# Two softmax products cut in halves, and weight blocks, softmax steps and loads at other places, in an attention, expert-FFN and routing kernel on one core

## The reference

```python
# attention: x (4, 8, 512, 64), state (4, 8, 32, 64)
scores  = scale * x @ state.T ;  a  = softmax(scores);   xread = a  @ state     # 512 rows a batch and head
scores2 = scale * state @ x.T ;  a2 = softmax(scores2);  sread = a2 @ x         # 32 rows a batch and head
x = concat([xread, sread], axis=2) -> (2176, 512)
# FFN: w_in (512, 2048), w_out (2048, 512)
h = x @ w_in ;  g = h * tanh(softplus(h)) ;  x = g @ w_out
# routing to 8 experts: logits = normalised x @ normalised expert_emb.T / tau
out[rows of expert e] = gate * (relu(x @ w1[e]) @ w2[e])
```

## Time and profile before

| | |
|---|---|
| median of three executions | 699.39 us (699.05 to 701.37) |
| the profiled execution: its own time | 701.31 us |
| the profiled execution: span, first to last instruction | 699.5 us |
| PE busy | 657.1 us, 94% of the span |
| DVE busy, ACT busy | 442.5 us, 385.9 us |
| granted PE clock, mean | 0.983 of full speed |

### The profile page before, as it was taken

How to read it: one execution, slowest core, us unless ns; L and a number is a source line. 1 busy time by engine, 2 the same in 40 slices (tenths; PEclk the granted TensorE clock), 3 DMA queues, 4 the chain that set the end, 5 groups by cost and what they waited for, 6 DMA issues and landing times.

```text
span 699.5 us, 12384 instructions
## 1 busy us (share of the span) xinstructions
PE 657.1 (94%) x4142; PEld 513.4 (73%) x4143; DVE 442.5 (63%) x687; ACT 385.9 (55%) x501; POOL 50.8 (7%) x75
## 2 busy tenths in 40 slices
PE   7889979999989999899999999889999999999995
PEld 5667657687767787676578877678888888888883
DVE  6899889979548699685677658462722452262261
ACT  2789678785547887477787453252622442261250
POOL 1000000000200002000000103001001010010101
PEclk9999999999989999999999999999999999999998
DMA  9713453000814000344000531472621360153140
GB/s 264 218 32 107 151 166 121 0 2 2 269 45 135 37 2 31 95 137 154 9 1 8 219 106 77 162 261 76 220 82 45 109 211 30 45 197 134 45 150 5
DMA packets 35350, 72.72 MB, mean 104 GB/s; under 512 B 5699, under 2 KB 5699, under 8 KB 35312
## 3 DMA queue, kind: packets, MB, share of 16 engines
q1 hardware_dynamic: 27728, 56.93, 25.3%
q0 software_dynamic: 3040, 9.13, 3.3%
q10 hardware_dynamic: 4544, 6.14, 2.9%
HBM read 60.92 MB, written 12.16 MB: 104 GB/s over the span
## 4 chain that ended last, share of the span: by engine, by line
PE 64%; DVE 16%; ACT 10%; issue 5%; DMA 4%; SPq 0%; ACTq 0%; POOL 0%; DVEq 0%; POOLq 0%
PE PS L708 16%; PE PS L736 16%; PE PS L613 11%; PE PS L569 7%; DVE ww L1384 3%; PE PS L717 3%; PE PS L524 3%; DMA raw<-in_w 2%; PE PS L478 2%; ACT ww L981 2%; DVE qq L1396 2%; ACT rr L977 2%; DVE qq L1379 2%; DVE gl L1402 2%; ACT rr L975 1%
## 5 line engine op out<-in xcount | busy, mean ns | idle before, releaser
L613 PE MATMUL PS<-WH,gh 128*128 128x512 f32 x256 | 103.3, 404 | 0.8 <-DVE gl L1402 0.8
L613 PE MATMUL PS<-WH,gl 128*128 128x512 f32 x256 | 101.0, 395 | 0.0
L613 PE MATMUL PS<-WL,gh 128*128 128x512 f32 x256 | 101.0, 394 | 0.0
L1067 ACT ACTIVATE hh<-PS 128x512 fp32r<-128x512 f32 x42 | 23.0, 596 | 96.4 <-PE PS L717 94.3
L736 PE MATMUL PS<-WH,hh 128*128 (+1 forms) x168 | 68.6, 409 | 3.1 <-DVE hl L1488 2.0
L1478 DVE TENSOR_TENSOR WL<-raw,WH 128x1024 f32 (+1 forms) x48 | 56.2, 1222 | 23.5 <-ACT WH L1047 23.4
L736 PE MATMUL PS<-WH,hl 128*128 (+1 forms) x168 | 66.5, 396 | 0.0
L736 PE MATMUL PS<-WL,hh 128*128 (+1 forms) x168 | 66.2, 394 | 0.0
L1379 DVE SCALAR_TENSOR_TENSOR qq<-ww,PS 128x1024 f32<-128x1024 f32 (+1 forms) x35 | 41.5, 1187 | 35.5 <-ACT ww L965 35.4
L981 ACT ACTIVATE ww<-ww,cst 128x1024 f32<-128x1024 f32 (+1 forms) x35 | 39.4, 1127 | 41.6 <-DVE ww L1384 41.6
L613 PEld LDWEIGHTS PS<-WH,gh 128*128 128x128 f32 x256 | 48.2, 188 | 18.8 <-issue 7.5
(11 more groups left out here) (252 smaller groups left out, 1281.8 us busy)
## 6 DMA issues: line engine op xcount, KB each, us to landing
raw<-in_w SPq DMA_DIRECT2D x48, 512.0 KB, 4.6
raw<-in_w_in SPq DMA_DIRECT2D x36, 512.0 KB, 4.9
yg<-by_expert ACTq DMA_DIRECT2D x22, 260.0 KB, 3.4
raw<-in_w_out SPq DMA_DIRECT2D x8, 512.0 KB, 4.6
by_expert<-junk SPq DMA_DIRECT2D x1, 2080.0 KB, 10.2
wr<-in_w_in SPq DMA_DIRECT2D x4, 512.0 KB, 9.4
x_0a<-in_x SPq DMA_DIRECT2D x8, 128.0 KB, 3.0
x_0b<-in_x SPq DMA_DIRECT2D x8, 128.0 KB, 3.6
```

The source lines that it names most:

```text
L613: mm = pe.matmul(PS[:, 2 + t, :], a[:, v % 2, e, t * P:t * P + P], w[:, 8 + p, e * 512:e * 512 + 512], start=(p == 0 and e == 0 and i == 0 ...
L1067: a.activation(hh[:, 4 * j:4 * j + 4, :], PS[:, 3 + j, :].rearrange("p (k m) -> p k m", k=4), ACT.Copy).then_inc(hh_rdy, 1)
```

## The change

It does six things.

1. `sread(1)`, `sread(2)` and `sread(3)` are cut in two: the products of t in `ahead` and `behind`, with the work of H or Y between the two halves. `sread(0)` stays whole.
2. In `sread(2)` and `sread(3)` the products of the two head groups g alternate, g = 1 writes a bank of its own (7) and another 32 partitions (q = j xor 1), so that eight parts of the array are used in turn instead of four. The reciprocal of the sums is written to the partitions that fit (five small DVE instructions instead of one), and `sread_out` needs two copies instead of four.
3. The blocks M(c+1, 1) and M(c+1, 2) of chunks 1 and 2 go to other pairs, M(c+1, 3) goes into the next chunk, and `M_hi`, `M_lo` with them, some of these between other steps of mish.
4. `scores_out`, `soft_1`, `soft_3`, `soft_4`, `exp_1` and `soft_5` of batches 2 and 3 go one pair or a few steps ahead.
5. In chunk 0, pair 5, ACT does `exp_1(1)` ahead of `sread_out(0)`, and `o_split(6)` behind the exponentials of mish.
6. In SP's queue `load_x(2)` goes behind four more weight loads, and `load_x(3)` behind four more.

```diff
             sp.dma_start(scr_v[0:PAD], ...).then_inc(zeros_out, 16)
+            for r in range(12, 16):
+                stream(r)
             load_x(2)
-            for r in range(12, RING["w", 2 * NB, 0]):
+            for r in range(16, RING["w", 2 * NB + 2, 0]):
                 stream(r)
             load_x(3)
...
-            def sread(b):
+            def sread(b, part):
                 pe.wait_ge(e2d_rdy, b + 1)
                 if b > 1:
-                    pe.wait_ge(m_lo, NB * b + 1)
+                    pe.wait_ge(m_lo, NB * b + 2)
...
+                order = [(g, t) for g in range(HG) for t in range(16)] if b < 2 else [(g, t) for t in range(16) for g in range(HG)]
+                for g, t in order[part]:
+                    for j in range(4):
+                        q = j if b < 2 else j ^ g
+                        mm = pe.matmul(PS[32 * q:32 * q + 32, sr_bank(b, g), D * g:D * g + D], E2D[b][32 * j:32 * j + 32, g, 32 * t:32 * t + 32],
+                                       X2[b % 2][t // 8][32 * j:32 * j + 32, g, t % 8, :],
+                                       start=(t == 0), stop=(t == 15))
+                if part.stop is None:
+                    mm.then_inc(sr_mm, 1)
...
+            whole, ahead, behind = slice(0, None), slice(0, 16), slice(16, None)
...
                     if p == 4:
+                        if c == 1:
+                            sread(1, behind)
                         route_k(c - 1)
+                    if p == 6:
+                        sread(c + 1, ahead)
+                    if p == 7:
+                        sread_turned(c + 1)
+                if c > 1 and p == 0:
+                    M(c, 3)
...
                     if p == 3 and c == 1:
-                        sread(1)
+                        sread(1, ahead)
                     if p == 5 and c > 0:
-                        sread(c + 1)
+                        M(c + 1, 1)
                     if p == 6 and c > 0:
-                        sread_turned(c + 1)
+                        sread(c + 1, behind)
                     if p == 7:
-                        M(c + 1, 3)
+                        M(c + 1, 3 if c == 0 else 2)
...
                 if u == 5:
+                    exp_1(1)
                     sread_out(0)
-                    exp_1(1)
-                    o_split(6)
...
-                if n == 4 and c in (1, 2):
+                if n == 3 and c in (1, 2):
                     exp_1(c + 1)
```

More of the change, by code:

```diff
@@ L267, in h_bank, with sr_bank, sh_upto, bv_upto @@
             return 6 if v == 1 else 0
+        def sr_bank(b, g):
+            return 6 if b < 2 else 6 + g
+        def sh_upto(b):
+            return (4, 8, 10, 12)[b]
+        def bv_upto(b):
+            return (2, 4, 10, 16)[b]
         def y_bank(t):
@@ L758, in _ @@
                     if p == 4:
-                        sread(0)
+                        sread(0, whole)
                 if c in (1, 2):
@@ L930, in sread_out @@
                 for h in range(2):
-                    for g in range(HG):
-                        a.activation(sh[D * h:D * h + D, 2 * g:2 * g + 2, NS * b:NS * b + NS], ps[:, g, :, h if g == 0 else 1 - h, :],
+                    if b < 2:
+                        for g in range(HG):
+                            a.activation(sh[D * h:D * h + D, 2 * g:2 * g + 2, NS * b:NS * b + NS], ps[:, g, :, h if g == 0 else 1 - h, :],
+                                         ACT.Copy).then_inc(sh_e, 1)
+                    else:
+                        a.activation(sh[D * h:D * h + D, :, NS * b:NS * b + NS].rearrange("p (g q) n -> p g q n", g=HG), ps[:, :, :, h, :],
                                      ACT.Copy).then_inc(sh_e, 1)
@@ L1085, in _ @@
                 mish_b(u)
+                if u == 6:
+                    o_split(6)
                 if u < PC - 1:
@@ L1120, in _ @@
                     mish_hi(u - 1)
+                if n == 7 and c in (1, 2):
+                    M_hi(c + 1, 1)
                 if done >= 0:
@@ L1140, in _ @@
                     exp_2(1)
+                if n == 6 and c in (1, 2):
+                    M_hi(c + 1, 0)
+                if n == 2 and c in (1, 2):
+                    scores_out(c + 1)
                 if done >= 0 and n == 1:
                     y_out(done)
+                    if c > 1:
+                        M_hi(c, 2)
                 mish_c(u)
+                if c == 1 and n == 0:
+                    M_hi(1, 2)
                 if done >= 0:
@@ L1326, in soft_5 @@
                 v.tensor_scalar(r2[:, b % 2, 2, :], r2[:, b % 2, 2, :], 1e-9, None, ALU.add).then_inc(bv, 1)
-                dve.wait_ge(bv, 2 * b + 1)
-                v.reciprocal(r2[:, b % 2, 3, :], r2[:, b % 2, 2, :]).then_inc(bv, 1)
+                if b < 2:
+                    dve.wait_ge(bv, bv_upto(b) - 1)
+                    v.reciprocal(r2[:, b % 2, 3, :], r2[:, b % 2, 2, :]).then_inc(bv, 1)
+                else:
+                    dve.wait_ge(bv, bv_upto(b) - 5)
+                    v.reciprocal(r2[:, b % 2, 3, 0:1], r2[:, b % 2, 2, 0:1]).then_inc(bv, 1)
+                    for j in range(4):
+                        q = j ^ 1
+                        v.reciprocal(r2[32 * q:32 * q + 32, b % 2, 3, 1:2], r2[32 * j:32 * j + 32, b % 2, 2, 1:2]).then_inc(bv, 1)
                 v.transpose(E2D[b][:], SC[:]).then_inc(e2d_rdy, 1)
@@ L1612, in _ @@
                     mish_lo(u - 1)
-                if kind == "m" and n < 3 and c > 0:
+                if n == 7 and c in (1, 2):
+                    M_lo(c + 1, 1)
+                if kind == "m" and (n in (0, 2) and c == 1 or n == 2 and c > 1):
                     M_lo(c, n + 1)
-                if n == 7 and c in (1, 2):
-                    M_lo(c + 1, 0)
                 if c == 1 and n == 0:
@@ L1624, in _ @@
                 mish_r(u)
+                if n == 6 and c in (1, 2):
+                    M_lo(c + 1, 0)
+                if n == 1 and c > 1:
+                    M_lo(c, 2)
                 if done >= 0 and n == 1:
@@ L1627, in _ @@
                 mish_g(u)
+                if n == 0 and c > 1:
+                    sread_scale(c)
+                if c == 1 and n == 0:
+                    M_lo(1, 2)
                 if c in (1, 2):
```

47 lines of the change are left out of this document (15 added, 32 removed).

## The result

Median 688.42 us over 4 runs (686.82 to 692.68), 700.38 us before on the same chip, 12.0 us less; the ratio is 0.985, 95% interval 0.981 to 0.989. The forecast was 686.9 us, range 683.5 to 691. The profiled execution took 686.94 us with a span of 685.2 us, of which PE was busy for 651.3 (95%); the forecast for it was a span of 687.0 us.

What follows compares the result with a forecast made beforehand. PE, busy 94% of the span, was taken as the bound, with time to win in idle and slow time at four places. 2.5 + 1.35 + 6.05 + 2.45 + 1.0 - 0.8 = 12.55 us, giving 686.9 us, range 683.5 to 691.

Steps and rivals of the forecast that it cites:

- Place 1: End of chunk 0: `exp_1(1)` first closes DVE's gap of 2.66 us ahead of H(8); 2.5 us won.
- Place 2: `sread(1)`: halves remove a 1.6 us hole in PE's instructions, less 0.25 for an extra trip; 1.35 us won.
- Place 3: End of chunk 1, around M(2,0), `sread(2)` and H(16): four things and an extra trip, sum 6.05 us won.
- (a): Place 3: weights of M(2,0) go before `load_x(3)` in SP's queue; 0.45 us won.
- (c): Place 3: `sread(2)` without a hole or a fall of the clock, instead of 7.11 us; 4.0 us won.
- (d): Place 3: an `M_lo` between `mish_e` and `mish_q` on DVE makes H(16) wait; 0.5 us lost.
- (b): Place 3: `sread(2)` no longer waits for `M_lo(2,0)`, which comes one pair earlier; 2.35 us won.
- Place 4: End of chunk 2: `sread(3)` loses its 1.05 us wait and 1.65 us hole, less 0.25; 2.45 us won.
- Eight places: `sread(2)` and `(3)`: matmuls 7 ns apart instead of 14, each product 1.8 us shorter; 0.5 each arrives, 1.0 us won.
- What ACT pays: Chunks 1 and 2: `exp_1` ahead of the mish steps at pair 3 delays `turned(1,1)`; 0.4 each, 0.8 us lost.
- Holes not cured: Rival: three holes of 1.65 us stay in the products, gain 7.6, 691.8 us; chance 0.08.
- DVE sets the pace: Rival: DVE's full list at chunk ends delays the next H or Y, some 3.5 us lost, 690.4 us; chance 0.16.

Runs made afterwards that it cites:

- e3_exp_behind: The changed kernel with ACT's `sread_out(0)` ahead of `exp_1(1)` again at the end of chunk 0; median 693.47 us.
- e4_halves_alone: The kernel before with one edit, the softmax products of batches 1, 2 and 3 in halves; median 698.75 us against 701.18, ratio 0.996.
- e1_whole: The changed kernel with the softmax products of batches 1, 2 and 3 run whole again; median 695.79 us.
- e7_exp_behind_b: The changed kernel with `exp_1(c+1)` behind `mish_b` instead of ahead of it in pairs 3 of chunks 1 and 2; median 687.09 us.
- e12_after_again: The changed kernel run once more, same code; median 688.0 us over five runs.
- e8_split_first: The kernel of e7_exp_behind_b with `sread(0)` in halves too, the second behind the first half of Y(4); median 688.48 us.

## Why the prediction was right, step by step

- **Place 1 (2.5).** The mechanism held: DVE's gap went and reached H(8) whole (2.70 in e3_exp_behind). Measured 3.30, 0.8 more than forecast. That the slow stretch behind H(8) costs nothing held only in part: it went with the wait, H(8) takes 2.93 instead of 4.49 us, and of the 1.56 us 1.31 were lost again at Y(8) as a wait for DVE's `y_out`, which is DVE's pace as I had it from the earlier trace rows.
- **Place 2 (1.35).** Right: 1.39 from the disappearance of the hole (41.00 against 42.39 in e4_halves_alone, 1.29 in e1_whole).
- **Place 3 (6.05).** With 0.5 for eight places 6.55, measured 7.08. Four places cost 0.89 there, so the rest is 6.2. The sum is near by errors that cancel, which is luck in part: step (a), the order of the loads, 0.45, is worth 2.49 once the second half of `sread(1)` comes an H later; step (c), put down to halves and a high clock, is worth 3.07 and not 4.0 (e1_whole, whose clock fell as well). The new wait (d), 0.5, is 0.32 of waiting in front of H(16). Step (b), the wait for `M_lo` of 2.35 us, is gone in the trace, but no run puts it back. The parts are not independent: halves without the loads and the moved blocks give 1.03 here.
- **Place 4 (2.45).** Right as a sum: with 0.5 for eight places and 0.98 for ACT, as measured, it would give 2.0; it gave 2.34. Its parts are less sure. The whole product costs 1.0 and not 1.4, and 1.05 for the wait, 1.0, 0.43 for eight places and -0.98 for ACT make 1.5 only. In the kernel after, PE waits 0.51 us at `sread_turned(3)`, so a longer product, put back alone, is hidden there in part.
- **Eight places (0.5 of 1.8 us each, 1.0).** The sum is right (1.27), by two errors that cancel: matmuls came 10.0 ns apart and not 7, so a product won 1.02 and not 1.8 us; but two thirds of it arrived. What M's row does not tell is how fast small matmuls can be handed out.
- **What ACT pays (0.8).** The place was right, `turned(1,1)` and its like; the size was not: 1.93 us (e7_exp_behind_b). The wait that the trace shows is 0.66 and 0.67, the loss 0.98 each; 0.11 of the rest is `route_l` itself, which takes 0.92 instead of 0.81 us behind the wait.
- **The rivals.** Holes not cured: excluded. DVE sets the pace: it does so by 1.31 us at Y(8), and by less at H(8) (0.94, of the 3.85 before), at H(16) (0.32) and at `sread_turned(3)` (0.51). More: the eight places did not arrive in full. One late stretch of half clock fewer than before (one, at 399.6 us, in place of two, apart from the last few us) is luck: e12_after_again, the same kernel, has twice the length at 399.2 us and one more at 675.7. Slower by drains: three trips more, and batch 1's balance of 1.39 leaves no room for 4 us each.
- **What would show it.** "Issue" once, no wait for `M_lo`, clock 1.00: seen. Matmuls 7 ns apart: not seen, 10.0. H(8) at 100.71 rather than 102, HB 14.0 us earlier rather than 12 (0.9 of it ahead of all four places), and a wait for DVE of over 1 us (Y(8), 1.31) that I had named as a sign of being wrong. It was one, for 1.3 us.
- **What is shown and what is not.** Put back one at a time, the halves cost 5.37 us, the exponential 3.90, the loads 2.80 and the eight places 1.27. That is 13.3 us, and 15.0 were won before ACT's loss of 1.93. The moved blocks and the earlier softmax steps have no run of their own; the two waits for `M_lo` that are gone were 3.4 us long, more than the 1.7 that are left, so the parts overlap.

## What to carry to other kernels

Count instructions, not only time: where many tiny matmuls follow each other, PE runs dry at positions fixed by the count from the program's start. Here 256 of its instructions had to last 3.0 to 3.7 us, so it helps to cut such a product into short pieces with slow work on both sides of each. A split that ends later moves everything that waits for its end; look at the load queues and at the readers of its PSUM bank behind that end before you price the split, and keep whole the piece that heads a chain. Where a step is put ahead in an engine's list, read who waits for the steps that now stand behind it, and put it behind those that are due. "Issue" in front of an instruction can be a semaphore that the profile did not match: look at what the engines that it depends on finished just before.

## What the runs showed that I had not expected

- From one hand-out limit to the next, 256 instructions on, it takes 3.0 to 3.7 us at all 19 holes in the traces. For one and the same place, `sread(0)`, it is 3.0 us in some runs and 3.7 in others (holes of 0.97 to 1.67 us). In each the instruction queue moves one packet of 16,384 bytes, and PE starts again 1.2 to 1.6 us behind it.
- Small matmuls with their weight loads came no faster than one in 8.7 ns in any run, with four parts in turn or with eight.
- A hole or wait of 1.3 to 1.9 us is followed by 3.4 us at half clock in some runs and not in others: a hole of 1.67 us in `sread(0)` was followed by none in the kernel before and by 3.4 us in e12_after_again. Waits of 3.64 and 3.70 us in front of H(8) (e3_exp_behind, e8_split_first) went with nearly 7 us of it each, while one of 3.67 us at the same place (e4_halves_alone) went with none. What decides it stays open.
- A trace without a fall of the clock repeats to 0.05 us over 220 us.
